# Attention steps taken in pairs inside a fused attention and MLP kernel on Trainium2

## The reference

```python
# q, k, v: (4, 8, 576, 64); 4 batches x 576 positions = 2304 tokens, 8 heads x 64 = 512 features
scores = where(0 <= i - j < 64, q @ k.T / 8, -1e9)
attn = exp(scores - max); attn = attn / (sum + 1e-9)
x = (attn @ v), heads side by side: (2304, 512)
# first MLP, 1536 wide
xn = x / sqrt(mean(x * x) + 1e-6) * rms_g
x = (silu(xn @ w_gate) * (xn @ w_val)) @ w_out
# second MLP, 2048 wide
h = x @ w_in
out = (h * sigmoid(1.702 * h)) @ w_out2
```

## Time and profile before

| what | value |
|---|---|
| median of 3 runs | 939.89 us (939.82 to 940.53) |
| the profiled execution, its time | 940.77 us |
| the profiled execution, its span | 938.8 us |
| PE busy | 926.7 us (99%) |
| PEld busy | 761.6 us (81%) |
| DVE busy | 351.2 us (37%) |
| ACT busy | 302.3 us (32%) |
| POOL busy | 144.2 us (15%) |
| share of the chain that ended last | PE 96%, DVE 2%, ACT 1%, issue 1% |
| q, k, v transfers, issue to landing | 2.2, 2.4, 2.7 us |
| mean granted TensorE clock | 0.998 |

### The profile page before, as it was taken

One profiled execution on the slowest core, in us unless ns is written; L12 is line 12 of the kernel. 1 busy time (PEld: TensorE's weight loads), 2 busy tenths in 40 slices (PEclk: granted clock), 3 DMA queues, 4 the chain that ended last, 5 costly groups with the idle time before them and its releaser, 6 DMA issues.

```text
span 938.8 us, 13531 instructions
## 1 busy us (share of the span) xinstructions
PE 926.7 (99%) x5324; PEld 761.6 (81%) x5324; DVE 351.2 (37%) x846; ACT 302.3 (32%) x726; POOL 144.2 (15%) x188
## 2 busy tenths in 40 slices
PE   8799999999999999999999999999999999999998
PEld 7699777787777877778888888888888888888897
DVE  6776523334233333323345552233224222322332
ACT  5555333343333433334111232232223222322232
POOL 5466121120211212122022210000000000000000
PEclk9999999999999999999999999999999999999999
DMA  8572221103220031100323230020002000200000
GB/s 264 178 221 79 72 59 52 34 1 95 59 62 23 1 102 53 35 2 1 134 90 103 99 113 1 0 65 26 1 1 89 1 1 1 68 1 0 29 17 23
DMA packets 33423, 52.91 MB, mean 56 GB/s; under 512 B 3408, under 2 KB 13648, under 8 KB 33360
## 3 DMA queue, kind: packets, MB, share of 16 engines
q1 hardware_dynamic: 32352, 50.61, 17.2%
q10 hardware_dynamic: 1008, 1.44, 0.4%
HBM read 42.60 MB, written 9.44 MB: 55 GB/s over the span
## 4 chain that ended last, share of the span: by engine, by line
PE 96%; DVE 2%; ACT 1%; issue 1%; POOL 0%; DVEq 0%; ACTq 0%
PE ps L527 24%; PE ps L529 22%; PE ps L528 22%; PE ps L671 7%; PE ps L672 7%; PE ps L673 7%; PE ps L512 2%; PE ps L477 2%; PE ps L497 2%; DVE w_all L915 1%; PE ps L597 0%; PE ps L524 0%; DVE sig L957 0%; POOL prob L385 0%; ACT h_hi L788 0%
## 5 line engine op out<-in xcount | busy, mean ns | idle before, releaser
L527 PE MATMUL ps<-x_hi,w_all 128*128 128x512 f32 (+1 forms) x800 | 302.4, 378 | 4.6 <-DVE w_all L915 3.3
L528 PE MATMUL ps<-x_hi,w_all 128*128 128x512 f32 (+1 forms) x800 | 295.2, 369 | 0.0
L529 PE MATMUL ps<-x_lo,w_all 128*128 128x512 f32 (+1 forms) x800 | 294.9, 369 | 0.0
L527 PEld LDWEIGHTS ps<-x_hi,w_all 128*128 128x128 f32 x800 | 150.9, 189 | 37.9 <-issue 10.2
L529 PEld LDWEIGHTS ps<-x_lo,w_all 128*128 128x128 f32 x800 | 151.2, 189 | 25.5
L528 PEld LDWEIGHTS ps<-x_hi,w_all 128*128 128x128 f32 x800 | 151.2, 189 | 23.8
L1027 DVE TENSOR_TENSOR hid<-ps,sig 128x512 f32<-128x512 f32 (+1 forms) x80 | 51.0, 638 | 207.8 <-ACT sig L829 207.5
L829 ACT ACTIVATE sig<-ps 128x512 f32<-128x512 f32 (+1 forms) x80 | 44.5, 556 | 215.5 <-PE ps L529 215.5
L671 PE MATMUL ps<-w_all,h_hi 128*128 128x512 f32 x288 | 112.2, 390 | 0.0
L672 PE MATMUL ps<-w_all,h_hi 128*128 128x512 f32 x288 | 112.2, 390 | 0.0
L673 PE MATMUL ps<-w_all,h_lo 128*128 128x512 f32 x288 | 112.0, 389 | 0.0
(11 more groups left out here) (91 smaller groups left out, 854.9 us busy)
## 6 DMA issues: line engine op xcount, KB each, us to landing
wstage<-in_w_a SPq DMA_DIRECT2D x36, 256.0 KB, 3.5
vwin<-in_v_win SPq DMA_DIRECT2D x33, 256.0 KB, 2.7
wstage<-in_w_b SPq DMA_DIRECT2D x32, 256.0 KB, 3.2
kwin<-in_k_t SPq DMA_DIRECT2D x32, 160.0 KB, 2.4
out_dram<-late SPq DMA_DIRECT2D x18, 256.0 KB, 2.1
qtok<-in_q_t SPq DMA_DIRECT2D x35, 128.0 KB, 2.2
xT<-x_scratch SPq DMA_DIRECT2D x4, 1024.0 KB, 5.3
x_scratch<-wstage SPq DMA_DIRECT2D x3, 1024.0 KB, 4.7
```

The source lines that it names most:

```text
L527: pe.matmul(out_, w[:, 0, cols], xh, start=first, stop=False, **flags)
L528: pe.matmul(out_, w[:, 1, cols], xh, start=False, stop=False, **flags)
L529: return pe.matmul(out_, w[:, 0, cols], xl, start=False, stop=last, **flags)
```

## The change

Steps go in pairs. In tile t, the pair for chunk 1, 3, 5 or 7 has both its scores at the end of that iteration; its four plus four transposes stand ahead of the projection two iterations later, and its value products behind that projection, directly ahead of the scores of the next pair. Value products move to bank 1 (`V_BANK`), which val uses too, scores of the two steps share banks 6 and 7, and the transposes of the two steps take one of these banks each. The ring has two slots. `sum_squares` moves behind the projection. The beginning is written in another order: no fillers between the first four scores, steps 2 and 3 load into tiles that are free at that time, `reciprocal_of_sum(0)` ahead of `row_max(2)`, two of the three low parts of the weights of chunk 2 ahead of the loop, and the loads of steps 4 and 5 behind the weights of chunk 2.

```diff
-    SLOTS = 3
+    SLOTS = 2
-    FIRST_STEP = 1
-    LAST_STEP = 8
+    SCORES_AT = (1, 3, 5, 7)
...
+    def pair_with_scores_at(t, c):
+        if t + 1 < NA and c in SCORES_AT:
+            return steps_of(t + 1)[0] + 2 * SCORES_AT.index(c)
+        return None
...
-            probT = sb("probT", [P, GB * P], F32, at)
+            probT = sb("probT", [P, 2, GB * P], F32, at)
...
         def scores_of(s, h):
-            bank = (4, 2, 0, 4)[s] if s < EARLY else 4 if s < steps_of(1)[1] else ATT_BANK
-            return ps[:, bank + h, 0:GT]
+            if s < EARLY:
+                return ps[:, (4, 2, 0, 4)[s] + h, 0:GT]
+            return ps[:, ATT_BANK + h, (s % 2) * GT:(s % 2 + 1) * GT]
 
         def pt_of(s):
-            return ps[:, (6, 2, 6, 2)[s] if s < EARLY else ATT_BANK + 1, :]
+            return ps[:, (6, 2, 6, 2)[s] if s < EARLY else ATT_BANK + s % 2, :]
 
         def o_of(s):
-            return ps[:, (7, 3, 7, 3)[s] if s < EARLY else ATT_BANK, 0:GT]
+            if s < EARLY:
+                return ps[:, (7, 3, 7, 3)[s], 0:GT]
+            return ps[:, V_BANK, (s % 2) * GT:(s % 2 + 1) * GT]
...
             def load_step_qk(s):
-                sp.wait_ge(scores_done, s - SLOTS + 1)
+                sp.wait_ge(scores_done, s - 1 if s >= EARLY + 2 else s - EARLY + 1)
...
-            load_step_qk(EARLY)
-            load_step_qk(EARLY + 1)
-            load_step_v(EARLY - 1)
-            load_step_v(EARLY)
             for m in range(3):
                 load_wA(2, m)
-            load_step_v(EARLY + 1)
+            for s in (EARLY, EARLY + 1):
+                load_step_qk(s)
+            for s in (EARLY, EARLY + 1):
+                load_step_v(s)
...
             def scores(s):
                 if s < EARLY:
                     wait(pe, max_ready, s - EARLY + 2)
-                else:
-                    pe.wait_ge(max_ready, s)
-                    if s in starts_of_tiles:
-                        pe.wait_ge(o_evacuated, s - EARLY)
-                    elif s > steps_of(1)[1]:
-                        pe.wait_ge(o_evacuated, s - 1 - EARLY)
+                elif s == EARLY:
+                    pe.wait_ge(early_squares, EARLY)
+                    pe.wait_ge(x_lo_ready, EARLY)
+                    pe.wait_ge(ln_done, 1)
+                elif s % 2 == 0:
+                    pe.wait_ge(probT_ready, s)
+                    pe.wait_ge(ln_done, home_of(s)[0])
...
-                    if s == EARLY:
-                        pe.wait_ge(early_squares, EARLY)
-                        pe.wait_ge(x_lo_ready, EARLY)
-                    else:
-                        pe.wait_ge(o_evacuated, s - EARLY)
-                    if s >= steps_of(1)[1] and s + 1 not in starts_of_tiles and s + 1 < STEPS:
-                        pe.wait_ge(max_ready, s + 2)
+                    pe.wait_ge(max_ready, s - s % 2 + 2)
...
-            def probs_by_v(s):
+            def probs_by_v(s, chunk=None):
...
-                elif s == EARLY:
-                    pe.wait_ge(ln_done, 1)
+                elif s % 2 == 0:
+                    pe.wait_ge(hidA_made, chunk + 1)
...
             def val(t, c):
...
+                multiplied = pair_with_scores_at(t, c - 3)
+                if multiplied is not None:
+                    pe.wait_ge(o_evacuated, multiplied + 2 - EARLY)
...
             for t in range(NA):
-                first, last = steps_of(t + 1) if t + 1 < NA else (0, 0)
                 for c in range(CA + LAG):
+                    scored = pair_with_scores_at(t, c)
+                    transposed = pair_with_scores_at(t, c - 2)
                     if c < CA and (t > 0 or c > 0):
                         gate(t, c)
                         if t == 0 and c == 1:
                             sum_squares(0)
-                        s = first + c - FIRST_STEP
-                        if first <= s < last:
-                            scores(s)
                         val(t, c)
-                    s = first + c - FIRST_STEP - 1
-                    if first <= s < last:
-                        transpose_probs(s)
-                    if c == SUMSQ_AT and last:
-                        sum_squares(t + 1)
+                    if transposed is not None:
+                        transpose_probs(transposed)
+                        transpose_probs(transposed + 1)
                     if c >= LAG:
                         project_A(t, c - LAG)
-                    if first <= s < last:
-                        probs_by_v(s)
+                    if transposed is not None:
+                        probs_by_v(transposed, CA * t + c)
+                        probs_by_v(transposed + 1)
+                    if scored is not None:
+                        scores(scored)
+                        scores(scored + 1)
+                    if c == SUMSQ_AT and t + 1 < NA:
+                        sum_squares(t + 1)
...
                 for c in range(CA):
-                    s = first + c - FIRST_STEP
-                    now = first <= s < last
+                    scored = pair_with_scores_at(t, c - 1)
+                    transposed = pair_with_scores_at(t, c - 2)
+                    multiplied = pair_with_scores_at(t, c - 3)
+                    if multiplied is not None:
+                        evacuate_o(multiplied)
+                        evacuate_o(multiplied + 1)
+                    if scored is not None:
+                        exponentials(scored)
                     tanh_A(t, c)
-                    if first <= s - 1 < last:
-                        copy_probT(s - 1)
+                    if scored is not None:
+                        exponentials(scored + 1)
+                    if transposed is not None:
+                        copy_probT(transposed)
+                        copy_probT(transposed + 1)
                     hid_hi_A(t, c)
...
                 for c in range(CA):
-                    s = first + c - FIRST_STEP
+                    scored = pair_with_scores_at(t, c - 1)
+                    if scored is not None:
+                        row_max(scored)
+                        row_max(scored + 1)
                     if t == 0:
                         scale_gate(c)
-                        if first <= s < last:
-                            row_max(s)
...
```

More of the change, by code:

```diff
@@ L111, in val_of @@
         def val_of(t, c):
[L112 removed]
+            return ps[:, 3 if t == 0 and c == 1 else V_BANK, 0:TILES_A[t][1]]
         def acc_of(t, j):
@@ L329, in _ @@
                             load_wA(c + 3, m)
-                    s = first + c - FIRST_STEP
-                    if first <= s < last and s + 2 < STEPS:
-                        load_step_qk(s + 2)
-                    s -= 1
-                    if first <= s < last and s + 2 < STEPS:
-                        load_step_v(s + 2)
+                    scored = pair_with_scores_at(t, c - 1)
+                    multiplied = pair_with_scores_at(t, c - 3)
+                    if scored is not None and scored + 2 < STEPS:
+                        load_step_qk(scored + 2)
+                        load_step_qk(scored + 3)
+                    if multiplied is not None and multiplied + 2 < STEPS:
+                        load_step_v(multiplied + 2)
+                        load_step_v(multiplied + 3)
                 store_x2(t)
@@ L431, in _ @@
             weights_hi_A(1, 1)
+            weights_hi_A(1, 2)
             add_early_square(2)
[L433 removed]
+            weights_hi_A(2, 0)
             add_early_square(3)
[L435 to L441 removed]
+            weights_hi_A(2, 1)
+            weights_hi_A(2, 2)
             for t in range(NA - 1):
[L444 removed]
                 for c in range(CA):
[L446 to L450 removed]
+                    scored = pair_with_scores_at(t, c - 1)
+                    multiplied = pair_with_scores_at(t, c - 3)
+                    for i in range(2):
+                        if multiplied is not None:
+                            squares(multiplied + i)
+                        if scored is not None:
+                            normalise(scored + i)
                     if t == 0 and c + 3 < CA:
@@ L453, in _ @@
                             weights_hi_A(c + 3, m)
+                    if t == 0 and c == 3:
+                        pool.wait_ge(early_sums, EARLY - 1)
+                        pool.wait_ge(w_hi_made, hi_madeA(c + 3, 1))
+                        pool.wait_ge(probs_normed, EARLY + 2)
+                        make_mask(2)
+                        pool.wait_ge(masks_made, 6)
                     if c == SUMSQ_AT:
@@ L751, in _ @@
             nc.scalar.preload_act_table_set(EXP_SET)
-            for s in range(1, SLOTS):
+            for s in range(1, EARLY):
                 load_v(act, s)
@@ L975, in _ @@
             for t in range(NA):
-                first, last = steps_of(t + 1) if t + 1 < NA else (0, 0)
                 for c in range(CA):
-                    s = first + c - FIRST_STEP
```

(22 more changed lines are left out.)

113 lines of the change are left out of this document (51 added, 62 removed).

## The result

Five runs of the changed kernel took 935.12 us (median, 934.79 to 936.07), five of the kernel before beside them 940.05 us: a ratio of 0.9945, interval [0.9934, 0.9957]. It is faster, as forecast, but by 4.9 us in place of 11.0. The time lies above the range of 923.5 to 933.5.

The account below looks back on a forecast made before the run. TensorE, with 96% of the chain that ends last, was taken as the bound. Tiles 1 to 3 (9.6 us) plus beginning and tile 0 (1.4) made 11.0 us off the median 939.89: 928.9 us, range 923.5 to 933.5.

Parts of the forecast that it names:

- Part 1: Pairs in tiles 1 to 3: fewer borders on TensorE, 3.2 us less per tile, 9.6 us in three.
- border: TensorE time lost entering and leaving a group of small matmuls: 0.31 us for value products, 0.38 for scores.
- mixed group: Two value products and two scores in a row on TensorE, in tiles 1 to 3 forecast at 2.37 us.
- inner step: Step from 128*64 to 64*64 inside a mixed group: taken as 0.18 us, bounds 0 and 0.38.
- Part 2: The beginning: TensorE's wait of 3.34 us goes, but it idles 3 us again; 1.4 us gain together with Part 3.
- Part 3: Tile 0: VectorE and ScalarE set a two-chunk loop of 12.8 us, within 0.2 of now; 1.4 us gain with Part 2.
- I add 0.6 for it: Tile 0's loop: 0.6 us added for VectorE's splits slowed beside POOL's normalise, making 12.8 us.
- upper bound of 13.8: Tile 0's longest loop in us: three splits at 1.35 each, less the 0.4 in which they have no company.
- B: Rival: tile 0 loses, with loops of 13.8 us and a cold clock for longer; 931.4 us, chance 0.12.
- A: Rival: tile 0 runs at TensorE's pace, saving 14.2 us in all; 925.7 us, chance 0.15.
- C: Rival: borders belong to each group of 16, not the shape change, so pairs keep them; 938.5 us, chance 0.05.
- D: Rival: TensorE is fed too slowly in a mixed group's 64 small matmuls; 964 us with nothing queued, chance 0.08.

Follow-up runs that it names:

- single_all: The changed kernel with all steps in all tiles taken one by one, leaving only the new beginning and two ring slots: 940.12 us.
- act_casts: The changed kernel with the high parts of the weights of chunks 5, 7, 9 and 11 all made on ScalarE, none on POOL: 930.83 us.
- pool_cut_tile0: The changed kernel with POOL's normalise and squares of steps 4 to 11 on 8 columns only, the rest left out: 928.31 us.
- cut_and_casts: The changed kernel with the edits of both act_casts and pool_cut_tile0 together: 925.8 us.
- single_tile0: The changed kernel with tile 0's steps 4 to 11 taken one by one as before, pairs kept in tiles 1 to 3: 927.58 us.
- single_tile0_again: The same program as single_tile0, run once more as a control on another experiment's chip: 928.21 us.

## Why the prediction was right and wrong

**Part 1** was right in its mechanism and nearly so in its numbers. The border is paid on leaving 128\*128 and coming back, once for two groups side by side. A mixed group costs 2.31 where I had 2.37, and a pair alone what I had. By the groups' records a tile of before spends 12.9 us on scores and value products (8 x 0.80 and 8 x 0.82) and 3.6 on transposes; a tile of after spends 3 x 2.32 + 1.28 + 1.24 = 9.5 and 3.5. That is 3.5 less where I forecast 3.2. The tile became 3.9 us shorter. The last 0.4 lies in the plain matmuls, 98.6 us before and 98.2 after, and I take it for what a border does to the matmuls behind the two that I counted; no run isolates it. The inner step was bounded rightly and taken too high: with the scores apart each group costs 0.26 more, so it is 0.06 to 0.12, not 0.18. That the array shape is what the border hangs on is argued, not shown: scores and value products also share that the trace has two records for each of their matmuls, where transposes and plain matmuls have one, and no run parts the two.

**Part 2** came as written: gate 3 idles 3 us (scale_gate at 34.97, forecast about 35), project waits for hidden (1). single_all shows the beginning alone to be worth nothing in the median.

**Part 3** is the step that failed, in its term "I add 0.6 for it". The loop was 14.0 to 14.8 us in place of 12.8 (14.57 and 14.48 from one start of row_max to the next), and even my upper bound of 13.8 was passed. I had counted that POOL works beside the first splits, but priced it by one row of a split beside one normalise, and ended POOL's work at 7.4 us with the normalise, although its two casts are queued behind it. Three splits of an even chunk take 3.55 us (my figure: 2.0 and 0.6), the low part ahead of them 0.94 in place of 0.42, the casts 2.09 in place of 1.17, and in odd chunks, for which I added nothing, the splits take 2.06 to 2.72. Per split it is 1.04 us on the mean of 18 against 0.675 before; 18 x 0.36 = 6.5 us of VectorE's time, not all of it on the path. act_casts and pool_cut_tile0 show that the loops shorten when this company goes, and cut_and_casts that with it gone the loop falls to TensorE's own 11.8. My 12.2 for the loop without company was therefore a fair sum, a little high; 0.6 stood where some 2 belonged.

The 7.0 us by which tile 1 starts late add up like this. The first row_max of the loops starts at 46.79, forecast 45.5: 1.3. The two loops behind it take 3.4 more than 25.6. From the last row_max (75.84) to the end of its value products (88.2) are 12.4 us, forecast 11.1: 1.3. Tile 1 starts 13.4 us behind them, forecast 12.4: 1.0, of which 0.6 was a wrong count and no loss, since the trace of before has 13.0 there as well. Half of the 7.0 is thus the two loops; the other parts hold slowed splits too (2.06 ahead of 46.79, 3.56 at 81.77), and the lower clock (0.88 in the third loop), which no run separates.

**The rivals.** B, tile 0 loses by the slowed split, was the one that happened, but with 931.4 us also priced too low: its loops of 13.8 were exceeded. A was wrong for this kernel; TensorE's pace came in cut_and_casts. C and D fell with the timeline above. The 62 ns per matmul of the Trainium skill, TensorE: Matmul & The Clock Gate, section "Wait — 56ns, not 53.3ns?", which I had put beside D, did not bind here: the group took 2.31 us where I had worked out an estimated 4.0 by them. That estimate also counted every record as a matmul. The trace has two records for each, 0.03 us apart, so a matmul of the kernel starts every 0.06 us in value products and every 0.053 in scores ((1.10 - 0.28) / 31 x 2), and by matmuls even that figure would have given 2.0 us. Whether the page's condition, hardware decode off, holds here is shown by no run.

**On the collision.** A split reads both operands from SBUF, as h_lo and the silu of tile 0 do, and all three grew beside POOL. The silu at 79.04 came 0.09 us behind a normalise of 1.04 us and took 1.24 in place of 0.42, so it ended 0.29 us behind the normalise, as if it had waited for it. Hidden (one operand in PSUM) stayed at 0.42 us and row_max (scores from PSUM) at 0.28, though POOL worked beside them. The Trainium skill, SBUF — State Buffer, section "Who interferes with whom", says so: a VectorE instruction with two SBUF inputs contends with a GpSimd instruction that reads SBUF, and the ports that the two engines share are an exclusive lock. The trace agrees in kind and nearly in size: three splits alone (1.89) and two casts alone (1.17) would take 3.06 us one after another, together they took 2.76. I priced the split by its row; what was missing is a count of all that POOL has queued there.

## What to carry to other kernels

Where two kinds of small matmul groups use array shapes other than that of the work around them, put them side by side: each excursion costs TensorE 0.3 to 0.4 us here, and having fewer of them gave 11.8 us in three tiles. Do it only where TensorE is the bound; where other engines keep pace by hand-over, lay their queues beside each other first, since VectorE work on two SBUF operands over POOL work costs both, and in tile 0 the order that staggers them was worth some 7 us, more than the pairs gave in any tile (3.9). The change done in three of its four places gave 927.6 us, done everywhere 935.1.

## What the runs showed of the hardware

- Both sides of a collision slow down, and casts do too: two casts 1.17 to 2.09 us, three splits 1.89 to 2.76 with casts alone beside them, 3.55 with a normalise as well.
- The cost of going from 128\*128 matmuls to a small group and back did not grow with the group: 0.31 us for 16 records of value products, 0.28 for 32. Value products straight to scores, 128\*64 to 64\*64, save 0.26 us against two excursions; the step between the two shapes costs 0.06 to 0.12.
- After TensorE's idle stretch of 3 us before gate 3 the granted clock fell to the level of 1.2 GHz for part of the next microseconds: 0.79 on the mean from 36 to 44 us (TensorE had been busy 3.1 of the 8 us before), with matmuls of 256 columns every 0.21 us at 36.43 where they start every 0.12 at the upper level. In single_tile0 one execution ran with a granted clock of 0.68 from 24 to 40 us and started tile 1 at 95.89, another (single_tile0_again) with 0.89 and started it at 93.75: the same program, 2.1 us apart.
